# Attention, routing and gated MLP in one program: softmax work put ahead of copies, ring items dealt out anew, row products and the last stores in smaller parts

## The reference

```
scores = q @ k.T / 8;  keep where scores >= max - tau, else -1e9
attn = softmax(scores);  x = attn @ v                     # heads joined: [4, 576, 512]
logits = x @ w_gate;  local = sigmoid(x @ w_local)
e[s] = argmax(logits[s]) if s == 0 or local[s] < 0.5 else e[s-1]
out[s] = softmax(logits[s])[e[s]] * relu(x[s] @ w1[e]) @ w2[e]
h = gelu(out @ w_in);  u, v = halves of h
v_n = (v - mean) / sqrt(var + 1e-6) * g_ln;  v_s = w_sg @ v_n + b_sg   # over the tokens
result = out + (u * v_s) @ w_out
```

## Time and profile before

| | |
|---|---|
| median of 3 runs | 971.12 us |
| profiled execution | 971.14 us, of which the span is 969.3 us |
| TensorE matmuls | 915.3 us busy, 94% of the span |
| VectorE | 557.6 us, 58% |
| ScalarE | 415.4 us, 43% |
| GpSimd | 378.1 us, 39% |
| chain that ended last | TensorE 52% of the span, VectorE 5%, DMA 3% |

### The profile page before, as it was taken

How to read it: one execution, slowest core, us unless ns; L and a number is a source line. 1 busy time by engine, 2 the same in 40 slices (tenths; PEclk the granted TensorE clock), 3 DMA queues, 4 the chain that set the end, 5 groups by cost and what they waited for, 6 DMA issues and landing times.

```text
span 969.3 us, 16335 instructions
## 1 busy us (share of the span) xinstructions
PE 915.3 (94%) x6071; PEld 772.3 (80%) x6071; DVE 557.6 (58%) x1208; ACT 415.4 (43%) x793; POOL 378.1 (39%) x344
## 2 busy tenths in 40 slices
PE   7899998999899998999999999999999999999996
PEld 6777887788778877788888887788869788897884
DVE  6777777777776745817854688460035445344352
ACT  4767666666666633333333333333323132031220
POOL 4344435544574241455655565554214023040100
PEclk7999999999999999999999999999999999999998
DMA  6322332232223014735655466430030020200101
GB/s 150 75 62 75 86 85 64 63 111 62 63 74 111 14 51 158 230 107 145 203 171 186 139 204 209 151 103 19 1 110 2 1 98 1 95 3 1 50 1 49
DMA packets 47709, 86.82 MB, mean 90 GB/s; under 512 B 8076, under 2 KB 16396, under 8 KB 47632
## 3 DMA queue, kind: packets, MB, share of 16 engines
q1 hardware_dynamic: 43632, 76.32, 26.6%
q0 software_dynamic: 4000, 9.45, 3.0%
HBM read 73.42 MB, written 15.99 MB: 92 GB/s over the span
## 4 chain that ended last, share of the span: by engine, by line
PE 52%; DVE 5%; DMA 3%; issue 1%; ACT 1%; DVEq 0%; POOLq 0%
PE ps_y L1432 4%; PE ps_y L1434 4%; PE ps_y L1433 4%; PE ps_a L1704 4%; PE ps_a L1706 4%; PE ps_a L1705 4%; PE ps_h L1393 4%; PE ps_h L1395 4%; PE ps_h L1394 4%; PE ps_v L1704 3%; DMA w_raw<-in_w 2%; DVE w_low L1326 2%; PE ps_v L1706 2%; PE ps_v L1705 2%; PE ps_r L1704 2%; PE ps_r L1705 2%
## 5 line engine op out<-in xcount | busy, mean ns | idle before, releaser
L822 DVE SCALAR_TENSOR_TENSOR probs<-ps_s,floor,expd 128x576 f32<-128x576 f32 x144 | 117.0, 812 | 61.6 <-ACT expd L469 61.1
L512 ACT COPY probs_t<-ps_ring 128x512 f32<-128x512 f32 (+1 forms) x192 | 105.9, 560 | 102.4 <-PE ps_ring L606 93.4
L558 PE MATMUL ps_s<-k_high,q_split 128*128 128x288 f32 x336 | 107.6, 338 | 13.3 <-DVE probs L822 10.0
L1318 DVE CAST w_high<-w_raw 128x1024 fp32r<-128x1024 f32 (+1 forms) x63 | 65.4, 1053 | 89.1 <-PE ps_h L1395 44.1
L469 ACT ACTIVATE expd<-ps_s,max_tau 128x576 f32<-128x576 f32 x144 | 108.0, 750 | 5.1 <-DVE max_tau L808 5.1
L808 DVE TENSOR_REDUCE max_tau<-ps_s 128x1 f32<-128x576 f32 x144 | 106.7, 741 | 0.3 <-PE ps_s L559 0.3
L637 PE MATMUL ps_ring<-probs_t,v_pair 128*64 128x144 f32 x1280 | 93.9, 295 | 3.6 <-ACT probs_t L512 3.6
L559 PE MATMUL ps_s<-k_low,q_split 128*128 128x288 f32 x336 | 93.0, 299 | 0.0
L558 PEld LDWEIGHTS ps_s<-k_high,q_split 128*128 128x128 f32 x336 | 65.0, 193 | 34.6 <-DVE probs L822 24.2
L1326 DVE TENSOR_TENSOR w_low<-w_raw,w_high 128x1024 fp32r<-128x1024 f32 x66 | 88.9, 1367 | 3.2 <-POOL ids L1192 3.2
L637 PEld LDWEIGHTS ps_ring<-probs_t,v_pair 128*64 128x64 f32 x1280 | 77.2, 139 | 14.7 <-ACT probs_t L512 7.1
(11 more groups left out here) (263 smaller groups left out, 2054.4 us busy)
## 6 DMA issues: line engine op xcount, KB each, us to landing
w_raw<-in_w SPq DMA_DIRECT2D x63, 512.0 KB, 4.1
k_in<-in_k SPq DMA_DIRECT2D x30, 288.0 KB, 4.2
q_in<-in_q SPq DMA_DIRECT2D x30, 288.0 KB, 4.2
v_pair<-in_v SPq DMA_DIRECT2D x16, 256.0 KB, 2.7
x_rows_dram<-scratch SPq DMA_DIRECT2D x4, 1024.0 KB, 4.6
out<-scratch SPq DMA_DIRECT2D x4, 1024.0 KB, 4.3
scratch<-in_dense SPq DMA_DIRECT2D x8, 384.0 KB, 5.5
scratch<-y_rows_dram SPq DMA_DIRECT2D x3, 1024.0 KB, 5.5
```

The costliest lines, as they stand in the source:

```text
L558: nc.tensor.matmul(out, lhs, k_high[par][:, h, cols], start=first, stop=False)
L822: nc.vector.scalar_tensor_tensor(out=row_of(pair, w).rearrange("p (a c) -> p a c", a=2), in0=scores(n), scalar=floor[:, n % 4:n % 4 + 1], ...
```

## The change

- `tails`, `last`, `sums` and `rest` get steps of their own (10, 11, 12 and 13 of their pair), so that a pair without routing has at most two items a step. Items of a step are ordered main, tails, last, sums, rest, then all others.
- The logits of a batch are two items (three tiles, then two) in place of five, and `early` is two items in place of one. The other routing items and VectorE's routing steps move; batch 2's last two `rows` items now stand in steps 150 and 152, after the last unit (143).
- ScalarE takes the exponential of a step before it copies the step's items; VectorE masks before it normalises the products with V. The scaling of q moves to units 0 and 2 (pair 0 keeps its places).
- Gated MLP: row tiles 0 and 1 wait chunk by chunk for the gated halves that they read; the transposes of the next batch stand behind row tile 1 (four tiles) and row tile 3 (the fifth), and VectorE's low parts likewise; the last batch is stored tile by tile.

```diff
-MAIN_AT, TAILS_AT, SUMS_AT, PV_AT = 3, W + 2, W + 4, W + 5
-LOGITS_AT, ROWS_AT = (15, 17, 19, 21, 24), (26, 28, 30, 33, 35)
-ARGMAX_AT, SPREAD_AT, CHOOSE_AT, CHOSEN_AT, PLACE_AT, IDS_AT = 26, 28, 32, 37, 38, 48
-WITHIN_AT = (42, 42, 39)
-SCALE_AT = (2, 3)
+MAIN_AT, TAILS_AT, LAST_AT, SUMS_AT, REST_AT, PV_AT = 3, W + 1, W + 2, W + 3, W + 4, W + 5
+LOGITS_AT, ROWS_AT = (15, 17), (22, 26, 33, 42, 44)
+ARGMAX_AT, SPREAD_AT, CHOOSE_AT, CHOSEN_AT, RANK_AT, PLACE_AT, IDS_AT = 20, 24, 32, 35, 37, 38, 49
+WITHIN_AT, RUN_AT, PROBS_AT = (43, 43, 39), (45, 45, 41), (47, 47, 43)
-LAST_EARLY_AT, LAST_SUM_AT, LAST_LOGITS_AT = 4, 10, (12, 13)
+LAST_EARLY_AT, LAST_SUM_AT, LAST_LOGITS_AT = (4, 6), 10, (12, 13)
...
+    order = ("main", "tails", "last", "sums", "rest")
+    for items in per_step:
+        items.sort(key=lambda item: order.index(item[0]) if item[0] in order else len(order))
...
         for n in steps:                                  # ScalarE
             pair, w = unit_of(n)
+            if n < UNITS:
+                exp_scores(n)
             for k, item in enumerate(STEPS[n]):
                 if item[0] not in BY_DVE:
                     evacuate(FIRST_OF_STEP[n] + k, item)
-            if n < UNITS:
-                exp_scores(n)
             for h in range(2):
-                if w == SCALE_AT[h] and pair + 1 < ALL_PAIRS:
+                if w == ((2, 3) if pair == 0 else (0, 2))[h] and pair + 1 < ALL_PAIRS:
                     scale_q(pair + 1, h)
...
                 row_max(n)                               # VectorE
+            if 0 < n <= UNITS:
+                mask(n - 1)
             if n > 0:
                 for k, item in enumerate(STEPS[n - 1]):
                     if item[0] == "pv":
                         pv_normalise(FIRST_OF_STEP[n - 1] + k, item)
-            if 0 < n <= UNITS:
-                mask(n - 1)
...
             elif kind == "logits":                       # TensorE, fill
-                r = rows(i)
-                for c in range(DC):
+                for t in LOGIT_TILES[i]:
+                    r = rows(t)
+                    for c in range(DC):
...
+            if last:                                     # SyncE, gated MLP
+                for t in range(QT):
+                    sp.wait_ge(row_out, QT * b + t + 1)
+                    sp.dma_start(batch_rows(io["out"], b, P * t, rows(t)), y[par][0:rows(t), t, :]).then_inc(stored, 16)
+                sp.wait_ge(stored, 32 * b + 16 * QT)
+                return
...
             gated_low(b, V_ITEMS - 1)                    # VectorE, gated MLP
-            if not last:
-                y_low(b + 1)
             for t in range(QT):
                 r = rows(t)
+                if not last and t == 2:
+                    y_low(b + 1, range(4))
+                if not last and t == 4:
+                    y_low(b + 1, range(4, QT))
...
-            if not last_batch:                           # TensorE, gated MLP
-                turn_y(b + 1, 1 - par)
             for t in range(QT):
+                if not last_batch and t == 2:
+                    turn_tiles(b + 1, 1 - par, range(4))
+                if not last_batch and t == 4:
+                    turn_tiles(b + 1, 1 - par, range(4, QT))
                 r = rows(t)
-                if t == 0:
+                pe.wait_ge(row_out, QT * b if t < 2 else QT * b + t - 1)
+                if t >= 2:
                     pe.wait_ge(gated_split, V_ITEMS * b + V_ITEMS)
-                    pe.wait_ge(row_out, QT * b)
-                elif t >= 2:
-                    pe.wait_ge(row_out, QT * b + t - 1)
                 for c in range(DC):
+                    if t < 2:
+                        pe.wait_ge(gated_split, V_ITEMS * b + 2 * c + 1)
+                        pe.sem_inc(passed, 1)
```

More of the change, by code:

```diff
@@ L72 @@
 SPAN = 2 * S + 2 * TAIL
-MAIN_AT, TAILS_AT, SUMS_AT, PV_AT = 3, W + 2, W + 4, W + 5
-LOGITS_AT, ROWS_AT = (15, 17, 19, 21, 24), (26, 28, 30, 33, 35)
-ARGMAX_AT, SPREAD_AT, CHOOSE_AT, CHOSEN_AT, PLACE_AT, IDS_AT = 26, 28, 32, 37, 38, 48
-WITHIN_AT = (42, 42, 39)
-SCALE_AT = (2, 3)
+MAIN_AT, TAILS_AT, LAST_AT, SUMS_AT, REST_AT, PV_AT = 3, W + 1, W + 2, W + 3, W + 4, W + 5
+LOGITS_AT, ROWS_AT = (15, 17), (22, 26, 33, 42, 44)
+ARGMAX_AT, SPREAD_AT, CHOOSE_AT, CHOSEN_AT, RANK_AT, PLACE_AT, IDS_AT = 20, 24, 32, 35, 37, 38, 49
+WITHIN_AT, RUN_AT, PROBS_AT = (43, 43, 39), (45, 45, 41), (47, 47, 43)
 START_FILLS = 16
-LAST_EARLY_AT, LAST_SUM_AT, LAST_LOGITS_AT = 4, 10, (12, 13)
-LAST_TILES = range(3), range(3, QT)
+LAST_EARLY_AT, LAST_SUM_AT, LAST_LOGITS_AT = (4, 6), 10, (12, 13)
+LOGIT_TILES = range(3), range(3, QT)
 LAST_ARGMAX_AT, LAST_CHOOSE_AT, LAST_PLACE_AT, LAST_IDS_AT = 14, 15, 16, 17
@@ L98, in step_items @@
             per_step[at + MAIN_AT + w].append(("main", w, p))
-        per_step[at + TAILS_AT] += [("tails", 0, p), ("last", 0, p)]
-        per_step[at + SUMS_AT] += [("sums", 0, p), ("rest", 0, p)]
+        per_step[at + TAILS_AT].append(("tails", 0, p))
+        per_step[at + LAST_AT].append(("last", 0, p))
+        per_step[at + SUMS_AT].append(("sums", 0, p))
+        per_step[at + REST_AT].append(("rest", 0, p))
     for b in range(last):
-        for i in range(QT):
+        for i in range(2):
             per_step[after_batch(b, LOGITS_AT[i])].append(("logits", i, b))
@@ L107, in step_items @@
             per_step[after_batch(b, SPREAD_AT)].append(("spread", i, b))
-        per_step[after_batch(b, CHOSEN_AT)] += [("chosen", 0, b), ("rank", 0, b)]
+        per_step[after_batch(b, CHOSEN_AT)].append(("chosen", 0, b))
+        per_step[after_batch(b, RANK_AT)].append(("rank", 0, b))
         if b < last - 1:
             per_step[after_batch(b, IDS_AT)].append(("ids", 0, b))
-    per_step[after_batch(last, LAST_EARLY_AT)].append(("early", 0, last))
+    for i in range(2):
+        per_step[after_batch(last, LAST_EARLY_AT[i])].append(("early", i, last))
     per_step[after_batch(last, LAST_SUM_AT)].append(("ids", 0, last - 1))
@@ L494, in evacuate @@
             elif kind == "logits":
-                r = rows(i)
-                out, src = logits[0:r, i, :], bank[0:r, 0:E + 1]
-            elif kind == "early":
-                nc.scalar.copy(logits[0:TAIL, FULL, :], bank[0:TAIL, FULL * (E + 1):QT * (E + 1)])
-                out, src = logits[:, 0:FULL, :], bank[:, 0:FULL * (E + 1)].rearrange("p (t e) -> p t e", t=FULL)
+                if i == 0:
+                    out, src = logits[:, 0:3, :], bank[:, 0:3 * (E + 1)].rearrange("p (t e) -> p t e", t=3)
+                else:
+                    nc.scalar.copy(logits[:, 3, :], bank[:, 3 * (E + 1):4 * (E + 1)])
+                    out, src = logits[0:TAIL, 4, :], bank[0:TAIL, 4 * (E + 1):5 * (E + 1)]
+            elif kind == "early":
+                if i == 0:
+                    out, src = logits[:, 0:3, :], bank[:, 0:3 * (E + 1)].rearrange("p (t e) -> p t e", t=3)
+                else:
+                    nc.scalar.copy(logits[:, 3, :], bank[:, 3 * (E + 1):4 * (E + 1)])
+                    out, src = logits[0:TAIL, 4, :], bank[0:TAIL, 4 * (E + 1):5 * (E + 1)]
             elif kind == "rows":
@@ L641, in fill @@
                     pe.wait_ge(dve_took, taken_from_ring("pv", PIECES - 1, PAIRS * of + PAIRS - 1))
-                r = rows(i)
-                for c in range(DC):
-                    last = nc.tensor.matmul(bank[0:r, 0:E + 1], x_t[of % 2][:, c, P * i:P * i + r], w_route[:, c, :],
-                                            start=(c == 0), stop=(c == DC - 1))
+                for t in LOGIT_TILES[i]:
+                    r = rows(t)
+                    for c in range(DC):
+                        last = nc.tensor.matmul(bank[0:r, (E + 1) * t:(E + 1) * (t + 1)], x_t[of % 2][:, c, P * t:P * t + r], w_route[:, c, :],
+                                                start=(c == 0), stop=(c == DC - 1))
             elif kind == "early":
                 pe.wait_ge(dve_took, taken_from_ring("pv", PIECES - 1, ALL_PAIRS - 2))
-                for t in range(QT):
+                for t in LOGIT_TILES[i]:
                     r = rows(t)
@@ L654, in fill @@
                 pe.wait_ge(dve_took, taken_from_ring("pv", PIECES - 2 + i, ALL_PAIRS - 1))
-                for t in LAST_TILES[i]:
+                for t in LOGIT_TILES[i]:
                     r = rows(t)
@@ L855, in add_late @@
             if i == 0:
-                dve.wait_ge(evacuated, out_of_ring("early", 0, B - 1))
+                dve.wait_ge(evacuated, out_of_ring("early", 1, B - 1))
                 nc.vector.tensor_tensor(logits[:, 0:3, :], bank[:, 0:3, :], logits[:, 0:3, :], ALU.add).then_inc(dve_took, 1)
@@ L864, in argmax @@
             if b < B - 1:
-                dve.wait_ge(evacuated, out_of_ring("logits", QT - 1, b))
+                dve.wait_ge(evacuated, out_of_ring("logits", 1, b))
             else:
@@ L997, in vector_steps @@
                         within_tiles(b)
-                    if n == after_batch(b, WITHIN_AT[b] + 1):
```

(7 more changed lines are left out.)

## The result

957.01 us (median of 4 runs, 954.79 to 958.54) against 969.98 (median of 4, 968.65 to 971.57): ratio 0.9864, 95% interval 0.9837 to 0.9891. The profiled execution took 956.94 us.

The account below looks back on a forecast made before the run. TensorE was taken to bound attention, with only its waits to be won. Attention's steps 16.0, its end 1.0 and the gated MLP 9.3 sum to 26.3 us: 971.1 - 26.3 = 944.8, so 945, range 937 to 956.

Parts of the forecast that it names:

- Bound and mechanism of plain pairs: Attention pairs without routing: TensorE bounds; need 18.3 us against 19.7, so at most 1.4 won; 1.2 taken.
- Scaling of q: Attention, ScalarE: scaling q earlier costs the same 2 x 0.7 us in other steps, inside its 6.3 idle.
- Routing: Pairs 5 to 15: 5.0 us of waiting per four pairs, 0.8 left; gains 4.2, 4.2 and 3.3 us.
- Rival 2, the clock: Three-tile logits items and transposes among row products bring the clock down: 10 us, so 955; chance 0.07.
- End of attention: Block's end: late store costs 1.2 us, low clock behind `early` goes (1.7), 0.5 of waits; net gain 1.0.
- Gated MLP: Waits between products, batch 3's idle, low clock, last store: 3.6 + 2.2 + 1.6 + 1.9 = 9.3 us gained.
- Rival 1: Attention: copies behind exponentials free ring banks later, their waits replace others; gains 8 us less, 953; chance 0.19.
- Rival 3: Attention: exponentials wait for VectorE's maxima, then copies and TensorE wait; 1.5 us a pair worse, 984; chance 0.05.

Follow-up runs that it names:

- experiment 12: Changed kernel with VectorE's argmax and chosen_probs chains back in their old steps, and q scaled in units 2 and 3 again: 940.4 us, ratio 0.9728.
- experiment 1: Changed kernel with VectorE's argmax chain of batches 0 to 2 and spread back at their old steps: 943.6 us, ratio 0.9767.
- experiment 2: Changed kernel with VectorE's chosen_probs chain of batches 0 and 1 back at its old step: 944.6 us, ratio 0.9775.
- experiment 9: Changed kernel with GpSimd's subtractions for k and q of pairs 7, 11 and 15 cut to one column: 937.4 us in a single run.
- experiment 7: Kernel before with only tails, last, sums and rest in steps of their own and the new item order: 967.8 us, ratio 0.9975.
- experiment 8: Kernel before with ScalarE's and VectorE's new orders and the dealing of tails, last, sums and rest: 953.0 us, ratio 0.9841.
- experiment 13: Changed kernel without the routing's part, whose items and VectorE steps stay as in the kernel before: 939.3 us, ratio 0.9699.
- experiment 3: Changed kernel with both VectorE chains, argmax and chosen_probs, back in their old steps: 932.8 us, ratio 0.9648.

## Why the prediction was wrong

- **Bound and mechanism of plain pairs: right, the size too small.** "At most its idle time can be won", 1.4, was the failing term: 2.5 were won. The need of 18.3 was summed with 0.53 per transposing item, the one value read, in front of a product with V. In front of scores the same item takes 0.36 (63.81 to 64.17 in the changed kernel), in front of another 0.43:

```profile
63.38 0.60 PE L618 MATMUL ps_ring<-ident,probs 128*128 128x128 f32 x4
63.81 0.60 PE L624 MATMUL ps_ring<-ident,probs 128*128 128x128 f32 x4
64.17 0.38 PE L570 MATMUL ps_s<-k_high,q_split 128*128 128x288 f32 x1
```

  In the kernel before it took 0.58 there (85.64 to 86.22), because the weight load of those scores waited for a mask. In a plain pair such weight loads waited 1.6 us in five waits, and 0.4 after the change (us in total, times, longest):

```profile
PEld ps_s L558 <- DVE probs L822: 1.6, 5, 0.6
...
PEld ps_s L570 <- DVE probs L835: 0.4, 2, 0.2
```

  TensorE's own idle column shows 0.36 of the 1.6, since a matmul's modelled end runs over the gap behind it. So the waits on masks were worth more than the 0.36 that the prediction gave them.
- **Scaling of q, costed at nothing ("inside its 6.3 idle"): wrong.** The move gains 0.5 us a pair. ScalarE's average idle time was no cover in the old place, the step in which two copies, an exponential and a scaling meet: in experiment 12 they keep ScalarE busy from 67.61 to 69.9 us, and TensorE's weight loads wait 0.8 us for copies in that pair against 0.2 with the scaling moved.
- **Routing: the step that failed.** "VectorE's chains (argmax, scan, probabilities) stay whole ... I leave 0.8 of the 5.0." The chains were costed at their old durations although they were moved to units 2 of their pairs, onto GpSimd's splits, whose times stood in the timeline. They cost 24.2 us (957.0 less 932.8; 21 by the ratios): up to the gated MLP's first product the change won 2.5 us where 17.0 were forecast. With them clear, attention gives about what was forecast and more: 932.8 against the 945.
- **Rival 2, the clock:** the low stretches came, six of them, but five go with the 2.7 and 3.6 us waits; one (110.4) goes with a logits item, as this rival had it, and none with the transposes. I had priced most of the symptom under another cause.
- **End of attention.** The store came last as forecast: TensorE waited 1.56 us in place of 0.48. The low stretch behind `early` is gone in this trace, but that is luck: in six of the nine traces with `early` in two items one begins in its first item or within 1 us behind it (at 335.9 with argmax back, for one), against five of six with one item. Behind the wait of 1.56 us, in seven of the eight traces that have it, stands another, which the prediction did not count; in the trace of the changed kernel neither came.
- **Gated MLP: right.** The row product follows after 0.22 us (753.49 to 753.71) in place of 3.5, no low clock in the last one (it had 0.50 in the earlier trace rows), 2.7 us after the last add where 3.2 were forecast. 11.7 in all against 9.3; 1.7 of the difference is a low stretch at 709.7 to 713.2 in the trace of before that the later one lacks.
- **Rival 1** did not come in the changed kernel: the masks' wait for exponentials fell from 61.1 to 2.2 us, and the copies cost TensorE almost nothing.
- **Rival 3** came in five places, though not in plain pairs: the exponentials' wait for row maxima rose from 5.1 to 23.2 us, 17 of them in front of the five waits of TensorE, where a maximum stood behind a held-up chain. Its mechanism was right for the routed pairs; the cause, slow chains, was not in it.

## What to carry to other kernels

When a block of small VectorE instructions is moved, look at what GpSimd does in the window it is moved to, not only at what waits for it: two-input instructions of 0.2 us became 1.05 to 1.36. Put the exponential ahead of copies and the mask ahead of results that wait for TensorE, and spread the fillings, but measure a dealt-out schedule chain by chain, since a wait of 3 us in the middle can cost as much again in clock. To bound a saturated engine, take start-to-start times for every pair of neighbours, as the idle column leaves out what overlap hides.

## What the runs showed of the hardware

VectorE's operations with two SBUF inputs wait for the GpSimd instruction in flight (here copies and subtractions that read SBUF), whatever their own size: 5 numbers a partition took 1.06 us, and 0.17 with GpSimd idle. Reductions (one input, 0.20) and the mask (one of its inputs in PSUM, 0.81) ran on beside it. The Trainium skill says this ("SBUF — State Buffer", two separate sides): VectorE and GpSimd share a port pair under an exclusive lock held for a whole instruction, taken by VectorE instructions with two SBUF inputs against GpSimd instructions that read SBUF. The traces agree, and the prediction should have used it. The Trainium skill's rule that transposes do not count as activity for the clock ("TensorE: Matmul & The Clock Gate", Part 4) had no effect that can be seen in the row products, which ran at 1.00 around 16 of them (753.7 to 765.0, the transposes from 759.3 to 760.9); no run here tests it further.

TensorE's clock fell to 1.2 GHz at waits of 2.7 to 3.6 us in the middle of otherwise full work, for 3.4 or 6.8 us: at all twelve of them in the changed kernel and experiments 1, 2 and 9. Of the six waits of 1.9 to 2.5 us in the middle of attention (experiments 7, 8 and 13) two had such a stretch behind them. Without such a wait it fell at 10 of the 24 logits items of three tiles, the one of 6.8 us at 273 us in experiment 3 among them. What decides where it did not fall is open.
